# Chunk 0's k turned on TensorE, its q and k loaded in two halves, and the last pair of chunks in another order

## What is computed

```python
# _attn_ref: q, k, v are (2, 8, 768, 64); lam has one decay for each head
for b in range(nb):                      # blocks of 64 positions
    intra = np.einsum('bhic,bhjc->bhij', qb, kb) * Dmask[None]   # lam ** (i - j) for i >= j
    intra = np.einsum('bhij,bhjd->bhid', intra, vb)
    inter = np.einsum('bhid,bhde->bhie', qb * lam_pow[None], kv_state)
    out[:, :, sl] = intra + inter
    kb_dec = kb * rev_pow[None]
    kv_state = lam_block * kv_state + np.einsum('bhsd,bhse->bhde', kb_dec, vb)
# _moe_ref on x = attention output (2, 768, 512), x_prev = x one position earlier
xk = mu_k * x + (1.0 - mu_k) * x_prev
xr = mu_r * x + (1.0 - mu_r) * x_prev
k = np.maximum(xk @ w_k, 0.0)            # 512 -> 1024
v = k * k @ w_v                          # 1024 -> 512
x2 = sigmoid(xr @ w_r) * v
# _moe2_ref on x2
gate = sigmoid(causal conv of 5 taps over x2)
out = (gate * (x2 @ w_val)) @ w_out
```

## Time and profile before

| | |
|---|---|
| median of 3 runs | 277.73 us (277.64 to 277.85) |
| the profiled execution | 277.8 us |
| its span | 276.0 us |
| TensorE matmuls busy | 269.2 us (98%), 1740 instructions |
| VectorE busy | 166.0 us (60%) |
| ScalarE busy | 125.4 us (45%) |
| GpSimd busy | 24.8 us (9%), all of it in the first 40 us |
| granted TensorE clock | 9 in tenths (full) in all 40 slices |
| loads in the first 41 us | 400 GB/s and more in most slices |

### The profile page before, as it was taken

How to read it: one execution, slowest core, us unless ns; L and a number is a source line. 1 busy time by engine, 2 the same in 40 slices (tenths; PEclk the granted TensorE clock), 3 DMA queues, 4 the chain that set the end, 5 groups by cost and what they waited for, 6 DMA issues and landing times.

```text
span 276.0 us, 4259 instructions
## 1 busy us (share of the span) xinstructions
PE 269.2 (98%) x1740; PEld 225.7 (82%) x1740; DVE 166.0 (60%) x257; ACT 125.4 (45%) x223; POOL 24.8 (9%) x26
## 2 busy tenths in 40 slices
PE   8889979999999999999999999999999999999996
PEld 7779967888888888888888888888888888888886
DVE  6766998999583123555886544438978599325000
ACT  2327786986782113456821143749217305412121
POOL 1857750000000000000000000000000000000000
PEclk9999999999999999999999999999999999999999
DMA  6999996000000000000000000440000000310323
GB/s 248 415 400 411 408 406 239 0 0 2 0 0 0 2 0 0 0 0 2 0 0 0 5 0 0 144 163 0 0 0 2 0 0 0 116 38 0 114 80 112
DMA packets 7506, 22.83 MB, mean 83 GB/s; under 512 B 960, under 2 KB 1216, under 8 KB 7488
## 3 DMA queue, kind: packets, MB, share of 16 engines
q1 hardware_dynamic: 7488, 22.57, 21.3%
HBM read 19.42 MB, written 3.15 MB: 82 GB/s over the span
## 4 chain that ended last, share of the span: by engine, by line
PE 85%; DVE 5%; DMA 4%; issue 2%; SPq 2%; ACT 1%; DVEq 0%
PE ps L703 28%; PE ps L704 28%; PE ps L705 28%; DMA qk<-in_qk 4%; DVE pT L508 2%; PE ps L774 1%; DVE xk_f L532 1%; DVE xk_l L538 1%; SPq L218 1%; SPq L223 1%; DVE state L525 1%; PE ps L758 0%; PE ps L719 0%; ACT x L330 0%; ACT faded L338 0%
## 5 line engine op out<-in xcount | busy, mean ns | idle before, releaser
L703 PE MATMUL ps<-xk_h,wk_h 128*128 128x512 f32 x96 | 37.6, 392 | 0.0
L704 PE MATMUL ps<-xk_l,wk_h 128*128 128x512 f32 x96 | 37.4, 389 | 0.0
L705 PE MATMUL ps<-xk_h,wk_l 128*128 128x512 f32 x96 | 37.3, 389 | 0.0
L703 PE MATMUL ps<-kk_h,wv_h 128*128 128x512 f32 x96 | 37.3, 389 | 0.0
L704 PE MATMUL ps<-kk_l,wv_h 128*128 128x512 f32 x96 | 37.3, 389 | 0.0
L705 PE MATMUL ps<-kk_h,wv_l 128*128 128x512 f32 x96 | 37.3, 389 | 0.0
L571 DVE SCALAR_TENSOR_TENSOR gate<-x,prm,gate 128x512 f32<-128x512 f32 x48 | 32.6, 744 | 0.0
L547 DVE SCALAR_TENSOR_TENSOR kk_f<-ps,ring 128x512 f32<-128x512 f32 x24 | 16.5, 688 | 24.4 <-ACT ring L367 24.4
L384 ACT ACTIVATE gate<-x,prm 128x512 f32<-128x512 f32 x12 | 8.7, 725 | 42.9 <-DVE x L557 42.9
L367 ACT ACTIVATE ring<-ps 128x512 f32<-128x512 f32 x24 | 14.3, 597 | 27.1 <-PE ps L705 27.1
L703 PEld LDWEIGHTS ps<-xk_h,wk_h 128*128 128x128 f32 x96 | 18.0, 188 | 4.1 <-issue 0.3
(11 more groups left out here) (71 smaller groups left out, 486.7 us busy)
## 6 DMA issues: line engine op xcount, KB each, us to landing
qk<-in_qk SPq DMA_DIRECT2D x12, 512.0 KB, 11.8
kv<-in_kv SPq DMA_DIRECT2D x10, 512.0 KB, 13.0
out<-out_sb SPq DMA_DIRECT2D x11, 256.0 KB, 2.0
wk_raw<-in_w_k SPq DMA_DIRECT2D x4, 512.0 KB, 14.3
wv_raw<-in_w_v SPq DMA_DIRECT2D x4, 512.0 KB, 12.4
wr_raw<-in_w_r SPq DMA_DIRECT2D x2, 512.0 KB, 14.7
w_raw<-in_w_val SPq DMA_DIRECT2D x2, 512.0 KB, 4.5
w_raw<-in_w_out SPq DMA_DIRECT2D x2, 512.0 KB, 7.0
```

What stands on the lines that cost most here:

```text
L703: nc.tensor.matmul(to, left(0), right(0), start=(i == 0), stop=False)
L704: nc.tensor.matmul(to, left(0), right(1), start=False, stop=False)
L705: done = nc.tensor.matmul(to, left(1), right(0), start=False, stop=(i == last))
```

## The change

It does four things. `kdec` of chunk 0 is no longer made by GpSimd from a token-major k: TensorE turns the feature-major k of chunk 0 with four transposes into PSUM bank 7 (`turn_k0`, behind `scores(1)`), and VectorE multiplies it by the decay into `kdec` (`decay_turned_k`, between `weigh(0)` and `om`). The load of kv of chunk 0 then has v alone. The host lays q and k so that two pairs of heads of both lie together, and chunk 0 comes as two transfers of 256 KB; `scores(0)` waits for each before its pairs, and `decay_q` reads q with a gap. In the last pair TensorE's order becomes `inter(10)`, `attend(10)`, `hidden(0, 0)`, `inter(11)`, `attend(11)`.

```diff
@@ SyncE
             def load_kv(n):
                 free(n)
-                first = 0 if has_update(n) else 1
+                first = 0 if has_update(n) and n > 0 else 1
...
             sp.dma_start(prm[:, :], prm_in).then_inc(prm_here, 16)
-            load_qk(0)
+            sp.dma_start(qk[0][:, 0:1, :, :], qk_in[0, :, 0:1, :, :]).then_inc(qk0_half, 16)
+            sp.dma_start(qk[0][:, 1:, :, :], qk_in[0, :, 1:, :, :]).then_inc(qk_here[0], 16)
@@ GpSimd
                     nc.gpsimd.tensor_tensor(
-                        qd[:, n % 4, :], qk[i][:, 0, :],
-                        qdec[:, :, :].rearrange("p a i -> p (a i)"), ALU.mult).then_inc(qd_ready, 1)
+                        qd[:, n % 4, :].rearrange("p (g c) -> p g c", g=2), qk[i][:, :, 0, :],
+                        qdec[:, :, :].rearrange("p (g a) i -> p g (a i)", g=2), ALU.mult).then_inc(qd_ready, 1)
...
             pool.wait_ge(dec_ok, H)
-            decay_k(0)
             pool.wait_ge(qdec_ok, PAIRS)
@@ VectorE
+            def decay_turned_k():
+
+                dve.wait_ge(k0_turned, 1)
+                nc.vector.tensor_tensor(
+                    kdec[:, 0, :].rearrange("p (r a d) -> p a r d", r=2, a=PAIRS),
+                    ps[:, TURNED, :].rearrange("p (a r d) -> p a r d", a=PAIRS, r=2),
+                    dec[:, :, CH - 1:CH].rearrange("p (r a) o -> p a r o", r=2).to_broadcast([P, PAIRS, 2, D]),
+                    ALU.mult).then_inc(kdec0_ready, 1)
...
             weigh(0)
+            decay_turned_k()
             nc.vector.tensor_scalar(om[:, :], prm[:, MU:MU + 2 * KT], -1.0, 1.0, ALU.mult, ALU.add).then_inc(om_ok, 1)
@@ TensorE
             def scores(n):
                 i = n % IN_BUFS
-                pe.wait_ge(qk_here[i], 16 * (n // IN_BUFS + 1))
+                if n > 0:
+                    pe.wait_ge(qk_here[i], 16 * (n // IN_BUFS + 1))
...
                 for a in range(PAIRS):
+                    if n == 0 and a == 0:
+                        pe.wait_ge(qk0_half, 16)
+                    if n == 0 and a == PAIRS // 2:
+                        pe.wait_ge(qk_here[0], 16)
...
+            def turn_k0():
+
+                pe.wait_ge(ident_ok, 1)
+                for a in range(PAIRS):
+                    cols = slice(a * P, (a + 1) * P)
+                    last = nc.tensor.transpose(ps[:, TURNED, cols], pair_of(0, 1, a), ident[:, :])
+                last.then_inc(k0_turned, 1)
...
             scores(0)
             scores(1)
+            turn_k0()
             attend(0)
...
                 inter(2 * p)
+                if p + 1 == NP:
+                    attend(2 * p)
+                    hidden(0, 0)
                 inter(2 * p + 1)
-                if p + 1 == NP:
-                    hidden(0, 0)
+                if p not in (OUT_FIRST, NP - 1):
+                    attend(2 * p)
                 if p != OUT_FIRST:
-                    attend(2 * p)
                     attend(2 * p + 1)
```

More of the change, by code:

```diff
@@ L35 @@
 CUTS = (0, 384, DM)
+TURNED = 7
 OUT_FIRST = 4
@@ L109, in build @@
         in_at = [kk_at + i * 8 * KB for i in range(4)] + [ring_at, r_at, wv_at + 16 * KB, wv_at + 24 * KB]
-        qk = [place(f"qk_{i}", [P, 2, DM], in_at[i]) for i in range(IN_BUFS)]
+        qk = [place(f"qk_{i}", [P, 2, 2, DM // 2], in_at[i]) for i in range(IN_BUFS)]
         kv = [place(f"kv_{i}", [P, 2, DM], in_at[i] + 4 * KB) for i in range(IN_BUFS)]
@@ L130, in build @@
         f32 = lambda z: z.bitcast(F32)
-        prm_here = sem("prm_here")
+        prm_here, qk0_half, k0_turned, kdec0_ready = [sem(z) for z in "prm_here qk0_half k0_turned kdec0_ready".split()]
         qk_here = [sem(f"qk_here{i}") for i in range(IN_BUFS)]
@@ L217, in load_qk @@
                 free(n)
-                sp.dma_start(qk[n % IN_BUFS][:, :, :], qk_in[n]).then_inc(qk_here[n % IN_BUFS], 16)
+                sp.dma_start(qk[n % IN_BUFS][:, :, :, :], qk_in[n]).then_inc(qk_here[n % IN_BUFS], 16)
             def load_kv(n):
                 free(n)
-                first = 0 if has_update(n) else 1
+                first = 0 if has_update(n) and n > 0 else 1
                 sp.dma_start(kv[n % IN_BUFS][:, first:, :], kv_in[n, :, first:, :]).then_inc(kv_here[n % IN_BUFS], 16)
@@ L709, in rows_of, with pair_of @@
                 return slice(row * D, (row + 1) * D)
+            def pair_of(i, of_k, a):
+                return qk[i][:, a // 2, of_k, a % 2 * P:(a % 2 + 1) * P]
             def scores(n):
                 i = n % IN_BUFS
-                pe.wait_ge(qk_here[i], 16 * (n // IN_BUFS + 1))
+                if n > 0:
+                    pe.wait_ge(qk_here[i], 16 * (n // IN_BUFS + 1))
                 if n >= 2:
@@ L716, in scores @@
                 for a in range(PAIRS):
+                    if n == 0 and a == 0:
+                        pe.wait_ge(qk0_half, 16)
+                    if n == 0 and a == PAIRS // 2:
+                        pe.wait_ge(qk_here[0], 16)
                     cols = slice(a * P, (a + 1) * P)
                     for row in range(2):
-                        last = nc.tensor.matmul(ps_s[n % 2][row][:, cols], qk[i][rows_of(row), 1, cols],
-                                                qk[i][rows_of(row), 0, cols], start=True, stop=True)
+                        last = nc.tensor.matmul(ps_s[n % 2][row][:, cols], pair_of(i, 1, a)[rows_of(row)],
+                                                pair_of(i, 0, a)[rows_of(row)], start=True, stop=True)
                 last.then_inc(scores_done, 1)
+            def turn_k0():
[4 more added lines that the diff above has]
+                last.then_inc(k0_turned, 1)
             def update(n):
@@ L729, in update @@
                 pe.wait_ge(kv_here[i], 16 * (n // IN_BUFS + 1))
-                pe.wait_ge(kdec_ready, u)
+                if n == 0:
+                    pe.wait_ge(kdec0_ready, 1)
+                else:
+                    pe.wait_ge(kdec_ready, u - 1)
                 if n >= 2:
@@ L952 @@
         "prm": prm,
-        "qk": np.stack([features(q), features(k)], axis=2),
+        "qk": np.stack([features(z).reshape(NCH, P, 2, DM // 2) for z in (q, k)], axis=3),
         "kv": np.stack([tokens(k[:, order]), tokens(v)], axis=2),
```

## The result

The changed kernel takes 278.65 us in the median of 22 runs (276.54 to 282.58), the kernel before 277.8 us in 22 runs beside it (277.45 to 278.54). The ratio is 1.0022, with a 95% interval of 1.0012 to 1.0033. This ratio and those further down average the runs within 1.5% of their kernel's fastest (here without 281.41 and 282.58), while the medians and ranges are of all runs. So it is slower by 0.2%. The forecast was 275.9, with a range of 275.5 to 276.8: wrong in sign.

What follows compares the result with a forecast made beforehand. The kernel was taken as bound by loads up to 17.79 us, then VectorE's chain, then a solid TensorE block from 47 us. Load 0.55 plus last pair 1.29 made 1.84: 277.73 - 1.84 = 275.9 us, range 275.5 to 276.8.

Steps and rivals of the forecast that it cites:

- qk of chunk 0 in two: At the head of the queue: splitting this load costs nothing, scores(1) still beginning at 6.00, or 6.04 with some loss.
- one of the signs that I had named: At scores(5): the forecast is wrong if they wait for TensorE; they should begin at 17.2 to 17.3, ended by DMA.
- The cover named, the scans: In the front: scans hold VectorE until weigh(0) at 6.52; without them the earlier first half is worth at most 0.20 us.
- The load, 0.55: Before scores(5): 256 KB less for kv of chunk 0 saves 0.55 us, ends 0.0 and 0.63.
- the saving holds for all later loads: In the load queue: all later loads come 0.55 us sooner, since the queue is issued 12 us ahead.
- The last pair, 1.29: Before inter(11): the new order gains 1.29 us of 1.63 idle, hidden(0, 1) at 45.68; ends 0.95 and 1.46.
- the wait for wk_l: Before hidden(0, 0) in the last pair: TensorE still waits 0.2 us for wk_l from VectorE.
- The turn: Behind scores(1): four transposes on TensorE take 0.88 us, ends 0.44 and 2.2, within a hole of 0.93 us.
- kdec(0): On VectorE after the turn: takes 0.65 us, ends at 8.9; update(0) begins 0.2 to 0.3 late.
- om: On VectorE before weigh(1): falls from 0.89 to 0.1 us once GpSimd's kdec(0) is gone from beside it.
- The front rival: Front, up to scores(5): transposes at 2.2 us make it late, 277.1; om still 0.89 gives 276.6; chance 0.16.
- The slower rival: Front work after the transposes: TensorE's clock falls to the 1.2 GHz level, scores(5) 8.2 late, 284.6 us; chance 0.04.

Runs made afterwards that it cites:

- kernel 7: The changed kernel with q and k of chunk 0 in one transfer and the old order of the last pair: 277.83 us, 1.0002 of the kernel before.
- kernel 1: The changed kernel with q and k of chunk 0 as one transfer again: 276.91 us, 0.9971 of the kernel before.
- 6: The changed kernel with q and k of chunk 0 in one transfer and kv of chunk 0 loaded whole: 277.39 us, 0.9979 of the kernel before.
- 10: The changed kernel with q and k of chunk 0 in one transfer, first loads issued only when the load four places ahead has landed: 277.09 us, ratio 0.9966.
- kernel 3: The kernel before with the new order of the last pair alone: 277.14 us, 0.9975 of the kernel before.
- 12: The kernel before with the new layout of q and k alone: 277.85 us, ratio 1.0001.
- 4: The changed kernel with kv of chunk 0 loaded whole, its k not used: 279.81 us, 1.0064 of the kernel before.
- kernel 9: The changed kernel with its first loads issued only when the load four places ahead has landed: 278.28 us, 1.0017 of the kernel before.
- 17: The changed kernel with q and k of chunk 0 in one transfer of 2 KB pieces, run once more: 279.74 us.
- 14: The changed kernel with q and k of chunk 0 in one transfer, but in pieces of 2 KB: 281.55 us, 1.0078 of the kernel before.
- 5: The kernel before with q and k of chunk 0 in two transfers of 64 partitions each, pieces still 4 KB: 278.79 us, ratio 1.0031.
- Kernel 8: The kernel before with the new layout and q and k of chunk 3 in two transfers: 278.62 us, 1.0024 of the kernel before.
- 13: The changed kernel with eight more warm-up matmuls between scores(0) and scores(1): 281.08 us, 1.0040 of the kernel before.
- 15: The changed kernel with eight more warm-up matmuls between scores(0) and scores(1), run once more for a profile: 281.03 us.

## Why the prediction was wrong

**The failed step: "qk of chunk 0 in two ... scores(1) still begins when qk of chunk 1 is there, 6.00 now, 6.04 with some loss. I cost it at nothing."** It begins at 8.07, 2.07 us late for a price of nothing, and so scores(5) wait for TensorE and not for their load, one of the signs that I had named. I had asked what is gained by a first half that lands early, and priced the loss by transfers deep in a full queue, at 0.4 us at most; I even put that loss under the load's saving rather than under scores(1), where 6.00 + 0.4 would have been 6.4; the 6.04 that I wrote follows from no row. At the head the same cut loses much more: landing 8.0 against 6.0, 198 GB/s against 397. Of the 2.0 us, 0.46 are a later issue, behind the one issue more (2.11 against 1.65), and 1.6 a longer way to landing (5.9 against 4.3). The cover named, the scans, hides a late scores(0) but not a late scores(1). The upper end should have come from the head's own rows.

**The load, 0.55, was not seen at the end.** Kernel 7 gives 0.0 +- 0.4 us; 1 and 6 differ by 0.2 us in the ratios and 0.5 in the medians, and so don't settle it. v of chunk 0 landed 5.1, 5.6 and 6.2 us after its issue in 10, 7 and 1, a whole kv 5.3, 5.9 and 6.3 us after it in the kernel before, 3 and 12. A rate measured in a full stretch doesn't price a transfer at the head. Nor did "the saving holds for all later loads" come true: chunk 5 landed 0.3 us earlier in kernel 1 and 0.2 later in kernel 7. Behind the head, one landing in each of these kernels comes 2.2 to 2.7 us after the one before it, where the other whole transfers follow at 1.2 to 1.6: chunk 4 in the kernel before (12.4 to 15.1), chunk 5 in 7 (15.5 to 18.0), chunk 7 in 1 (20.7 to 22.9). So the idle of 0.84 us before scores(5), which the term was to shorten, hung on where this late landing fell.

**The last pair, 1.29, was right as a length and wrong as a gain.** It measures 7.57 - 6.20 = 1.37 in the changed kernel and 1.38 in kernel 3, without the wait for wk_l. What I missed is that the idle time of 1.63 us was also slack. In the old order inter(11) waits for VectorE's state, so that TensorE may be late, as kernel 7 showed with 0.87 us at no cost. With the idle filled, every lateness ahead of inter(10) goes to the end. Kernel 3's inter(10) was 0.49 late, the changed kernel's 2.42.

**The sum by rows.** Forecast for hidden(0, 1): 46.97 - 1.84 = 45.13. Measured: 48.02, 2.89 later. scores(5) were to start at 17.24 and start at 19.17: 1.93. From there to inter(10) I had 21.61 us as before, and it is 22.65: 1.04. Of these, 0.31 are loads of two inters (1.17 against 0.86), 0.42 and 0.21 are the two idles named "issue" (0.74 and 0.71 against 0.32 and 0.50), and 0.10 are small differences. The pair is 6.20 and not 6.28: -0.08. Together 2.89.

**What held.** The turn is one instruction for each transpose, 0.42 us of loads and 0.66 of matmuls, below the 0.88 taken, and kdec(0) takes 0.69 against 0.65. The Trainium skill ("TensorE: Matmul & The Clock Gate", Part 4) gives about 275 ns for one bf16 transpose within a kernel, and an estimate from it was 1.1 us for four; the trace has 0.66 us for four float32 ones, each 0.29 us long and overlapping. The granted clock stayed 1.00 behind the turn in kernel 1 and in the changed one, so the rival that went by the same section of the Trainium skill (transposes do not count as busy time) did not come true here; four transposes between matmuls are a small test of it. The clock did fall in some runs (4, 9, 17), behind an idle wait and not behind transposes. om takes 0.16 and not 0.89 once GpSimd's kdec is gone from beside it, and 1.03 where the next kdec falls beside it: as the Trainium skill has it ("SBUF — State Buffer", "SBUF: two separate sides"), and the trace agrees in both directions. The block from hidden(0, 1) on has the same length.

**The rivals.** None of them was this one. The front rival had the right place, but its price came from the transposes and it ended at 277.1. The slower rival had the clock as its cause, where the split's landing was the cause and the clock a follower.

**The best version** is kernel 1, the change with q and k of chunk 0 in one transfer: 276.91 us, 0.9971 of the time before. The order alone (3) has nearly all of that, 0.9975; paced, the two read 0.9966 and 0.9969. The intervals overlap, so none of the four is shown to be faster than the others.

## What stays open

Why the head of the queue is so touchy is not settled. Smaller pieces (14) and a second transfer (5) each make chunk 0 whole at 5.9 to 6.0 us and chunk 1 at 7.2 to 7.4; the split by heads has chunk 0 whole at 4.8 to 5.5 and chunk 1 mostly at 7.7 to 8.2, so it may not be the same thing. Transfers from kv 1 on running ahead are excluded by the pacing (9), the layout by 12. What the queue does in its first microseconds wasn't seen. Also open are the idles of TensorE named "issue", 0.7 us each in the changed kernel and in 1 and 6 at the same places of the program, 0.3 to 0.5 in the kernel before, and another of 0.39 us in kernel 3. They take 0.6 us more than those of the kernel before, and the releaser column names nothing for them. The DMA view points at something. Beside the loads it has a queue named "instruction", whose packets of 16 KB take about 1.1 us each and come every 6 to 7 us. Its row in the window from 12 to 13.5 us of the kernel before (packets, MB, share of 16 engines):

```profile
q8 instruction: 1, 0.02, 4.5%
```

In the changed kernel such packets start at 29.23 and 36.20, and the two idles end at 31.72 and 38.77. In the 19 profiles TensorE has 37 idles of 0.25 us and more in the middle of a step's loads between 8 and 50 us that no DMA or state explains, and each ends 2.35 to 2.62 us after such a packet has begun. So TensorE most likely waits there for its own instructions; no run changed their number to test it. The late landings named above, chunk 4 before, 5 in 7 and 7 in 1, also fall right behind such a packet (12.38, 15.13 and 20.72 us), but not every packet has one: the changed kernel has none behind 16.09. Kernel 8's profiled run (278.13 us) has hidden(0, 1) at 47.32, 0.35 us late, with scores(5) 0.58 late. That is about half of the loss of 0.24% (0.66 us); the rest, and why chunk 5 was late, are open.

## What to carry to other kernels

Price a change to the first loads of a queue from landings at its head, not from the full rate further on, and look at who needs the *next* transfer rather than the one that is split. Before an idle time is filled, ask how much lateness it absorbs: once it is filled, every late wait ahead of it reaches the end. When several small edits are made together, time each alone: here one edit alone cost 1.5 us, another alone gained 0.7, and of a third no gain could be told.

## What was unexpected of the hardware

- A transfer of 512 KB in 128 pieces of 4 KB at the head of the queue had landed by 4.74 us. With pieces of 2 KB (14), or cut by partitions (5), it was whole at 5.9 to 6.0. Cut by heads into halves of 2 KB pieces it was whole at 5.5, in time for its matmuls, and the next transfer was 2 us late.
- The DMA share read 0.90 to 1.03 in stretches that moved 198 as well as 397 GB/s: a full share at the head says nothing of bytes.
- One and the same kernel ran in 277 or 281 us at full clock (13, 15), and what differed in the two profiles was which instructions of VectorE and GpSimd met: xk_l took 754 or 1432 ns.
- In the first 10 us, 16 weight loads took 1.5 to 1.8 us instead of 0.97, at the pace of the lower level, in stretches where the view by stretch shows a granted clock of 1.00 (the changed kernel at 4.90) as well as 0.52 (kernel 9 at 8.20). So the loads' own length is the better reading there.
- TensorE's idles in the middle of a step ended 2.35 to 2.62 us after a 16 KB packet of the queue named "instruction" had begun, in all 19 profiles.
